# The low part of the values made ahead of the diagonal's sum, in a linear-attention and mixture-of-experts kernel

## The chip, the cores and the metric

The kernel runs on one core of a Trainium2 chip. Time is the device time of one execution in microseconds (us), as the median of some runs. The core's engines are TensorE (PE in the rows, its weight loads PEld), VectorE (DVE), ScalarE (ACT), GpSimd (POOL) and SyncE (SP), which here issues the DMAs. Each engine works through its own queue in order and meets the others at semaphores.

## The reference

Three stages follow each other: a linear attention with decay over 768 positions, a gated two-layer network, and a soft mixture of experts. Cut to what matters:

```python
for t in range(S):                                   # B, H, S, D = 4, 8, 768, 48
    cur = einsum('bhd,bhe->bhde', u[None] * k_t, v_t)
    y[:, :, t] = einsum('bhd,bhde->bhe', r_t, state + cur)
    state = w_t[..., None] * state + einsum('bhd,bhe->bhde', k_t, v_t)
x = y.transpose(0, 2, 1, 3).reshape(B * S, H * D)    # 3072 x 384
h = x @ w_in                                         # 384 -> 2048
x = (h * clip(h + 3, 0, 6) / 6) @ w_out
logits = x @ phi                                     # 32 slots
slots = softmax(logits over tokens).T @ x            # then 8 experts: relu(slots @ w1) @ w2
out = softmax(logits over slots) @ slots_out
```

## The kernel before

The attention is cut into 24 units of 128 positions: six chunks, and in each the four batches (unit n has batch n % 4). Within a unit the decayed sum over earlier positions of the same chunk is a masked product of scores and values, and what comes from earlier chunks goes through `state`. The term with `u` concerns each position alone: the sum over d of r * k * u for each of the 8 heads (`diag`, 128 x 8) times v.

The gated network runs over 96 steps: six groups of 512 tokens (one chunk of all batches) with 16 pieces of 128 hidden columns. A step s is nine matmuls of 128x512 in half precision on TensorE (`mlp`, L568 to L570), a relu on ScalarE (L1343), and on VectorE the gate (L997) and a transpose (L1018). `mlp(s)` needs gate s - 2. The steps are at the same time the clock of the attention: every unit has four of them, called phases 0 to 3, and `unit_of(s)` gives `divmod(s + 19, 4)`. The first five units are in part done ahead of the loop; units 5 to 23 have their phases in it. The order on each engine is written out by hand in that engine's loop, and nothing reorders it.

Values and scores are split into a high and a low half-precision part, so that TensorE can multiply them in half precision. For one unit n these are the pieces that matter here:

- ScalarE makes `v_hi` in phase 0 (`high_v`, L1273); VectorE makes `v_lo` = 64 * v - `v_hi` in phase 2 (`low_v`, L981, 128x384, both inputs in SBUF). TensorE's `attend` in phase 3 (L534 first, then L540 to L544) waits for it, and so does SyncE's load of the unit that takes the same buffer.
- GpSimd makes r * k * u in phase 0 (`diag_products`, L1494 and L1496); VectorE sums it by heads in phase 2 (`sum_diag`, L977, 128x384 to 128x8); GpSimd's `diag_values` (L1517) in phase 3 multiplies it with v, and `finish_y` (L955) on VectorE adds that to the output of `attend`. The next unit's `diag_products` waits for `diag_done` too.
- VectorE's `mask_scores` (L936) and `scan_suffix` (L904) in phase 1, `low_x` (L970) in phase 2 (for every fourth unit in phase 1), `scan_prefix` (L916) in phase 3. GpSimd's `low_scores` (L1523) in phase 1, `decay_keys` (L1532) in phase 2, `decay_receptance` (L1541) in phase 3, behind `scan_prefix`. TensorE's `score` (L470) in the next phase 0 needs both. In the first steps of the loop GpSimd also makes the low part of w_in (`low_w`, L1508), twice per unit in units 5 to 7.

On VectorE, phase 2 in the loop is followed by the gate and the transpose of the same step.

Of the kernel before, what the change touches and what calls it, by code (L numbers as in the profile page):

```python
# [48 lines left out]
def build_program(nc, wT, rkT, nat_in_dram, u, u_blocks, w_in, w_outT, w_out, phi, w1, w2, out):  # L49
    with ExitStack() as ctx:  # L50
# [14 lines left out]
        def pairs(ap, n):  # L65
            return ap.rearrange("p (i n) -> p i n", n=n)
# [88 lines left out]
        def nat_of(n, which):  # L155
            return nat_rows_of(n)[:, which * DM:(which + 1) * DM]
# [54 lines left out]
        def by_slot(ap):  # L211
            return ap.rearrange("p (i s) -> p i s", s=SLOTS)
# [128 lines left out]
        def unit_of(s):  # L341
            return divmod(s + 4 * B + 3, 4)

        def is_unit(n):
            return 0 <= n < UNITS
# [551 lines left out]
        def _(dve):  # L897
# [35 lines left out]
            def mask_scores(n):  # L933
                dve.wait_ge(scores_ready, 2 * n + 2)
                dve.wait_ge(scores_lo_done, n - B)
                nc.vector.tensor_tensor(scores.rearrange("p (o n) -> p o n", o=PB),  # L936
                                        sc_ps[:, :].rearrange("p (o n) -> p o n", o=PB),
                                        mask[:].rearrange("p (o n) -> p o n", o=1).broadcast_to([P, PB, 2 * P]),
                                        ALU.mult).then_inc(masked, 2)
# [10 lines left out]
            def finish_y(n):  # L950
                dve.wait_ge(y_ready, n + 1)
                dve.wait_ge(diag_v_done, n + 1)
                if n:
                    dve.wait_ge(x_turned, n)
                nc.vector.scalar_tensor_tensor(y_nat, y_ps[:, 0:DM], 1.0 / (Y_SCALE if n >= B else SCORE_SCALE), diag_v,  # L955
                                               ALU.mult, ALU.add)\
                    .then_inc(y_done, 1)

            def add_state(n):
                dve.wait_ge(inc_ready, 2 * n + 2)  # L960
                for j in range(2):
                    rows = slice(ALIGN * j, ALIGN * j + D)
                    s = state[n % B][rows, :, j * D:(j + 1) * D]
                    new = pairs(inc_ps[rows, 0:PB * 2 * D], 2 * D)[:, :, j * D:(j + 1) * D]
                    last = nc.vector.tensor_tensor(s, s, new, ALU.add)
                last.then_inc(state_added, 1)
# [6 lines left out]
            def sum_diag(n):  # L973
                dve.wait_ge(rku_done, n - B + 1)
                if n:
                    dve.wait_ge(diag_v_done, n)
                nc.vector.tensor_reduce(diag[:], pairs(rku, D), AX_X, ALU.add).then_inc(diag_done, 1)  # L977

            def low_v(n):
                dve.wait_ge(v_hi_done, n - B + 1)  # L980
                nc.vector.scalar_tensor_tensor(v_lo[n % 2], nat_of(n, 2), V_SCALE, v_hi[n % 2],  # L981
                                               ALU.mult, ALU.subtract).then_inc(v_lo_done, 1)
# [10 lines left out]
            def gate(s):  # L993
                dve.wait_ge(relu_done, s + 1)
                if s >= GATED:
                    dve.wait_ge(l_ready, 4 * ((s - GATED) // 4 + 1))
                nc.vector.scalar_tensor_tensor(gated_tile(s), relu_tile(s), 6.0 * GATE, hid[s % 2][:],  # L997
                                               ALU.min, ALU.mult).then_inc(gated_done, 1)
# [10 lines left out]
            def turn_gated(s):  # L1009
                g, i = divmod(s, FT)  # L1010
                dve.wait_ge(gated_done, s + 1)
                if s == STEPS - 1:
                    dve.wait_ge(late_gated_done, 1)
                if i >= 4 and g:
                    dve.wait_ge(dg_ready, 16 * g)
                elif g >= 2:
                    dve.wait_ge(dg_ready, 16 * (g - 1))
                nc.vector.transpose(ring_tile(s), gated_tile(s)).then_inc(gated_turned, 1)  # L1018
# [5 lines left out]
            def group_maximum(g):  # L1024
                dve.wait_ge(folded, g + 1)
                if g >= 2:
                    dve.wait_ge(alpha_done, g - 1)
                nc.vector.tensor_reduce(group_max, l_ps[:], AX_X, ALU.max).then_inc(group_max_done, 1)
                dve.wait_ge(group_max_done, g + 1)
                lower(group_max, g).then_inc(neg_max_done, 1)  # L1030
# [108 lines left out]
            for s in range(END):  # L1139
                n, phase = unit_of(s)  # L1140
                g, i = divmod(s, FT)
                if s <= 1:
                    gate(s)
                    if s == 0:
                        low_v(B)
                    turn_gated(s)
                if phase == 0:
                    if is_unit(n - 1):
                        finish_y(n - 1)
                    if n - 1 < LAST_INC:  # L1150
                        add_state(n - 1)
                if phase == 1:
                    if 1 <= g < C and i == 2:
                        group_maximum(g - 1)
                    if is_unit(n):
                        mask_scores(n)
                    if is_unit(n + 1):
                        scan_suffix(n + 1)
                        restart_prefix(n + 1)
                    if is_unit(n - 1) and n % B == 0 and n > B:  # L1160
                        low_x(n - 1)
                    if 1 <= g < C and i == 2:
                        if g == C - 1:
                            turn_gated(s - 1)
                        turn_weight(g - 1)
                        turn_logits(g - 1)
                    if g == C and i == 2:
                        last_maximum()
                if phase == 2:
                    if g == C and i == 3:  # L1170
                        turn_weight(C - 1)
                    if g >= 1 and i == 3:
                        sum_weight(g - 1)
                    if is_unit(n - 1) and n % B:
                        low_x(n - 1)
                    if is_unit(n):
                        sum_diag(n)
                        low_v(n)
                if s == 0:
                    sum_diag(B)  # L1180
                    low_w(1)
                if phase == 3:
                    if is_unit(n + 1) and n > B:
                        scan_prefix(n + 1)
                    if s == STEPS + 4:
                        dve.wait_ge(run_sum_done, C)
                        nc.vector.tensor_scalar(run_sum, run_sum, 1e-9, None, ALU.add).then_inc(sum_inv_step, 1)
                        dve.wait_ge(sum_inv_step, 1)
                        nc.vector.reciprocal(run_sum, run_sum).then_inc(sum_inv_step, 1)
                        dve.wait_ge(sum_inv_step, 2)  # L1190
                        nc.vector.tensor_scalar(fold_inv[:], fold32, run_sum, None, ALU.mult).then_inc(fold_inv_done, 1)
                        dve.wait_ge(fold_inv_done, 1)
                        nc.vector.tensor_scalar(fold_alpha, fold_inv[:], alpha, None, ALU.mult).then_inc(fold_inv_done, 1)
                    if 1 <= g < C and i == 4:
                        add_slots(g - 1)
                if s == 4:
                    dve.wait_ge(w_phi_ready, 4)
                    nc.vector.transpose(w_phi[:], l_ps[:]).then_inc(w_phi_done, 1)
                if s == STEPS - 12:
                    cols, tiles = c_parts[0]  # L1200
                    dve.wait_ge(logits_done, C - 1)
                    nc.vector.tensor_reduce(cmax[:, tiles], by_slot(soft[:, cols]), AX_X, ALU.max).then_inc(c_max_done, 1)
                if s == STEPS - 8:
                    c_inverse(0)
                if s == STEPS + 3:
                    copy_cT(1)
                    copy_cT(0)
                if 1 < s < STEPS - 1:
                    gate(s)
                if 1 < s < STEPS - 2 and s != STEPS - FT + 1:  # L1210
                    turn_gated(s)
                if s == STEPS - 1:
                    last_gate(0)
                    turn_gated(STEPS - 2)
                    last_gate(1)
                    turn_gated(STEPS - 1)
# [462 lines left out]
```

## Time and profile before

| | us |
|---|---|
| median of 3 runs (lowest to highest) | 422.92 (421.85 to 425.69) |
| profiled execution, its own time | 421.91 |
| its span | 420.2 |
| VectorE busy in it | 338.0 |
| GpSimd busy in it | 187.7 |

The span is the time from the first to the last instruction of the profiled execution; its own time has what lies around that as well. TensorE's granted clock was 0.992 of full speed in the mean. A start time in a row counts from the span's start. TensorE's matmuls are pipelined and overlap, so that one which is listed with 0.38 us is followed by the next after 0.22.

### The profile page before, as it was taken

What the parts mean: (1) busy time and instruction counts of PE and PEld (TensorE: products, weight loads), DVE (VectorE), ACT (ScalarE), POOL (GpSimd) and SP (SyncE); (2) the same over time, 40 slices, a digit from 0 to 9 for tenths busy, and PEclk for the clock granted to TensorE, in tenths of its full rate; (3) what the DMA queues carried; (4) which work ended last, traced back from release to release, by engine and by line L of the source; (5) the groups of instructions that cost most, each with busy time, mean ns of one, the idle gap of its engine ahead of it and who ended that gap; (6) DMA issues with size and microseconds to landing.
All of it is one profiled execution on the core that took longest, in us unless ns stands there. A gap on an engine that the chain in (4) does not pass through costs nothing.

```text
span 420.2 us, 9784 instructions
## 1 busy us (share of the span) xinstructions
PE 402.2 (96%) x3914; PEld 220.2 (52%) x3914; DVE 338.0 (80%) x559; ACT 162.3 (39%) x297; POOL 187.7 (45%) x178
## 2 busy tenths in 40 slices
PE   8999999999999999999999999989999999999981
PEld 3884555555555555555555555445553444543430
DVE  7998799998998988989989988989875787661151
ACT  3586256534334244244343333341433234421141
POOL 4445988874555654455744557454540012010000
PEclk9999999999999999999999999999999999999996
DMA  8998331368034213304340331231007099879929
GB/s 245 354 400 277 123 96 29 123 264 274 11 122 122 80 48 123 116 9 123 124 123 2 123 120 51 77 123 58 0 4 297 4 367 411 247 272 420 386 97 357
DMA packets 16397, 69.35 MB, mean 165 GB/s; under 512 B 2144, under 2 KB 2912, under 8 KB 14688
## 3 DMA queue, kind: packets, MB, share of 16 engines
q1 hardware_dynamic: 16352, 68.73, 46.5%
q8 instruction: 31, 0.51, 0.5%
q14 instruction: 14, 0.11, 0.1%
HBM read 64.00 MB, written 4.72 MB: 164 GB/s over the span
## 4 chain that ended last, share of the span: by engine, by line
issue 35%; PE 29%; POOL 22%; DMA 5%; DVE 4%; ACT 1%; POOLq 0%; SPq 0%; DVEq 0%
POOL att L1532 5%; PE hid L568 4%; PE hid L570 4%; DMA att<-rkT_dram 4%; PE hid L569 4%; POOL att L1494 4%; POOL att L1496 4%; POOL att L1517 3%; POOL att L1550 3%; POOL w_split L1508 3%; PE hid L834 3%; PE l_ps L675 2%; PE hid L815 1%; PE sc_ps L815 1%; PE l_ps L615 1%
## 5 line engine op out<-in xcount | busy, mean ns | idle before, releaser
L1343 ACT ACTIVATE relu<-hid,three 128x512 f32<-128x512 f32 x95 | 65.2, 686 | 138.0 <-PE hid L570 137.7
L568 PE MATMUL hid<-x_split,w_split 128*128 128x512 f16 x285 | 108.3, 380 | 0.4 <-DVE gated L997 0.4
L570 PE MATMUL hid<-x_split,w_split 128*128 128x512 f16 x285 | 108.0, 379 | 0.0
L569 PE MATMUL hid<-x_split,w_split 128*128 128x512 f16 x285 | 108.0, 379 | 0.0
L997 DVE SCALAR_TENSOR_TENSOR gated<-relu,hid 128x512 f32<-128x512 f32 x95 | 64.4, 678 | 22.8 <-ACT relu L1343 22.1
L1018 DVE STREAM_TRANSPOSE ring<-gated 128x512 f32<-128x512 f32 x96 | 68.3, 711 | 3.3
L1523 POOL TENSOR_TENSOR att<-att 128x1024 f16<-128x1024 f32 x20 | 40.9, 2045 | 48.4 <-ACT att L1278 48.4
L1541 POOL TENSOR_TENSOR att<-att 112x512 f32<-112x512 f32 x19 | 23.2, 1220 | 57.0 <-DVE att L916 57.0
L568 PEld LDWEIGHTS hid<-x_split,w_split 128*128 128x128 f16 x285 | 27.7, 97 | 36.8 <-DVE gated L997 6.3
L570 PEld LDWEIGHTS hid<-x_split,w_split 128*128 128x128 f16 x285 | 27.8, 98 | 33.7
L569 PEld LDWEIGHTS hid<-x_split,w_split 128*128 128x128 f16 x285 | 27.9, 98 | 25.0 <-issue 0.3
L534 PE MATMUL y_ps<-att 112*128 112x96 f32 x160 | 33.6, 294 | 2.0 <-DVE att L981 1.4
L1532 POOL TENSOR_TENSOR att<-att 112x512 f32<-112x512 f32 x21 | 25.8, 1229 | 9.6 <-DVE att L904 9.6
L470 PEld LDWEIGHTS sc_ps<-att 48*128 48x128 f32 x384 | 23.3, 187 | 10.7 <-issue 10.7
L904 DVE TENSOR_TENSOR_SCAN att<-att 112x517 f32<-112x517 f32 x22 | 27.9, 1269 | 1.2 <-DMA att<-wT_dram 1.2
L916 DVE TENSOR_TENSOR_SCAN att<-att 112x517 f32<-112x517 f32 x22 | 28.2, 1284 | 0.0
L534 PEld LDWEIGHTS y_ps<-att 112*128 112x128 f32 x160 | 24.9, 189 | 6.4 <-issue 4.6
L470 PE MATMUL sc_ps<-att 48*128 48x128 f32 x384 | 27.9, 284 | 0.0
L1301 ACT ACTIVATE x_split<-y_ps 128x384 f16<-128x384 f32 x24 | 11.8, 491 | 41.1 <-PE y_ps L551 41.1
L675 PE MATMUL l_ps<-ring,soft 32*32 32x512 f32 x192 | 25.4, 593 | 2.3 <-DVE logits L1037 1.5
L675 PE MATMUL sc_ps<-ring,soft 32*32 32x512 f32 x384 | 26.1, 598 | 0.0
L1278 ACT ACTIVATE att<-att 128x1024 f16<-128x1024 f32 x20 | 21.1, 1057 | 11.6 <-DVE att L936 10.9
(269 smaller groups left out, 757.7 us busy)
## 6 DMA issues: line engine op xcount, KB each, us to landing
att<-nat_dram SPq DMA_DIRECT2D x20, 576.0 KB, 4.0
att<-rkT_dram SPq DMA_DIRECT2D x22, 448.0 KB, 5.5
att<-wT_dram SPq DMA_DIRECT2D x22, 226.2 KB, 4.7
att<-w_dram SPq DMA_DIRECT2D x3, 1536.0 KB, 10.0
out_dram<-w_split SPq DMA_DIRECT2D x12, 384.0 KB, 3.9
att<-w_dram SPq DMA_DIRECT2D x5, 768.0 KB, 9.9
stage<-w_in_dram SPq DMA_DIRECT2D x2, 1536.0 KB, 13.6
ring<-w_outT_dram SPq DMA_DIRECT2D x1, 3072.0 KB, 15.2
```

Of the source, the lines that this page charges most:

```text
L470: last = pe.matmul(sc_bank[j][:, cols], k_dec[n % 2][rows, cols], r_dec[n % 2][rows, cols], start=True, stop=True)
L534: pe.matmul(both, r_dec[n % 2][0:PD, p * P:(p + 1) * P], state[b][0:PD, p, :], start=True, stop=False, skip_group_check=True)
L568: pe.matmul(hid[s % 2][:], high, x_high, start=(q == 0), stop=False)
L569: pe.matmul(hid[s % 2][:], high, x_low, start=False, stop=False)
L570: last = pe.matmul(hid[s % 2][:], low, x_high, start=False, stop=(q == KT - 1))
L675: ins = pe.matmul(dg_bank[a][SLOTS * c:SLOTS * (c + 1), :], weight_T[SLOTS * a:SLOTS * (a + 1), b * SLOTS:(b + 1) * SLOTS], ring_group(g, ...
L916: nc.vector.tensor_tensor_scan(prefix[0:PD, :], w_rows_of(n)[0:PD, :], restart[0:PD, :], 1.0, ALU.mult, ALU.add).then_inc(prefix_done, 1)
L997: nc.vector.scalar_tensor_tensor(gated_tile(s), relu_tile(s), 6.0 * GATE, hid[s % 2][:], ALU.min, ALU.mult).then_inc(gated_done, 1)
L1018: nc.vector.transpose(ring_tile(s), gated_tile(s)).then_inc(gated_turned, 1)
L1343: nc.scalar.activation(relu_tile(s), hid[s % 2][:], ACT.Relu, bias=three[:], scale=GATE / H_SCALE)\
L1523: nc.gpsimd.tensor_tensor(scores_lo, scores, scores_hi, ALU.subtract).then_inc(scores_lo_done, 1)
L1532: nc.gpsimd.tensor_tensor(dst, keys, decay, ALU.mult).then_inc(k_dec_done, 1)
```

## The change

In phase 2 of each unit of the loop, on VectorE, `low_v(n)` stands ahead of `sum_diag(n)` in place of behind it. Both functions, their waits and their signals are as before. The unit whose pair lies ahead of the loop's phase 2 (unit 4) is not touched.

```diff
                     if is_unit(n - 1) and n % B:
                         low_x(n - 1)
                     if is_unit(n):
+                        low_v(n)
                         sum_diag(n)
-                        low_v(n)
                 if s == 0:
                     sum_diag(B)
```

On VectorE in phase 2 of unit 6, between the transpose of the step before and the next `scan_prefix` (L970 is `low_x`, L977 `sum_diag`, L981 `low_v`, L997 the gate, L1018 the transpose, L916 `scan_prefix`). Before:

```order
L970 SCALAR_TENSOR_TENSOR x_split<-y_ps,x_split 128x3x128
L977 TENSOR_REDUCE diag<-att 128x8
L981 SCALAR_TENSOR_TENSOR att<-att 128x384
L997 SCALAR_TENSOR_TENSOR gated<-relu,hid 128x512
L1018 STREAM_TRANSPOSE ring<-gated 128x512
L916 SCALAR_TENSOR_TENSOR att<-att 112x517
```

And in the changed kernel:

```order
L970 SCALAR_TENSOR_TENSOR x_split<-y_ps,x_split 128x3x128
L981 SCALAR_TENSOR_TENSOR att<-att 128x384
L977 TENSOR_REDUCE diag<-att 128x8
L997 SCALAR_TENSOR_TENSOR gated<-relu,hid 128x512
L1018 STREAM_TRANSPOSE ring<-gated 128x512
L916 SCALAR_TENSOR_TENSOR att<-att 112x517
```

`low_v` now follows `low_x`, and `sum_diag` stands between it and the gate.

In a unit whose number is a multiple of four (here unit 8) `low_x` is further ahead, in phase 1, and the pair follows a gate and a transpose (L936 `mask_scores`, L904 `scan_suffix`, L909 a reciprocal). Before:

```order
L936 TENSOR_TENSOR att<-sc_ps,mask 128x1024
L904 SCALAR_TENSOR_TENSOR att<-att 112x517
L909 RECIPROCAL att<-att 112x4
L970 SCALAR_TENSOR_TENSOR x_split<-y_ps,x_split 128x3x128
L997 SCALAR_TENSOR_TENSOR gated<-relu,hid 128x512
L1018 STREAM_TRANSPOSE ring<-gated 128x512
L977 TENSOR_REDUCE diag<-att 128x8
L981 SCALAR_TENSOR_TENSOR att<-att 128x384
L997 SCALAR_TENSOR_TENSOR gated<-relu,hid 128x512
```

And in the changed kernel:

```order
L936 TENSOR_TENSOR att<-sc_ps,mask 128x1024
L904 SCALAR_TENSOR_TENSOR att<-att 112x517
L909 RECIPROCAL att<-att 112x4
L970 SCALAR_TENSOR_TENSOR x_split<-y_ps,x_split 128x3x128
L997 SCALAR_TENSOR_TENSOR gated<-relu,hid 128x512
L1018 STREAM_TRANSPOSE ring<-gated 128x512
L981 SCALAR_TENSOR_TENSOR att<-att 128x384
L977 TENSOR_REDUCE diag<-att 128x8
L997 SCALAR_TENSOR_TENSOR gated<-relu,hid 128x512
```

`low_v` here comes straight behind the transpose. The queues of TensorE, ScalarE, GpSimd and SyncE are the same in both kernels.

## Rows read from the trace of the kernel before

**Rows 1.** The page's head: span; busy us (share of the span) xinstructions.
```profile
span 420.2 us, 9784 instructions
PE 402.2 (96%) x3914; PEld 220.2 (52%) x3914; DVE 338.0 (80%) x559; ACT 162.3 (39%) x297; POOL 187.7 (45%) x178
```

**Rows 2.** Lines L981 and L977 by source: shortest/median/longest ns, first to last start.
```profile
L981 DVE SCALAR_TENSOR_TENSOR att<-att x20: 543/706/1440, 39.6 to 311.0; 128x384 f16<-128x384 f32 x20
L977 DVE TENSOR_REDUCE diag<-att x20: 504/532/544, 40.9 to 310.5; 128x8 f32<-128x384 f32 x20
```

**Rows 3.** Waits: who <- for whom: us in total, times, longest.
```profile
DVE gated L997 <- ACT relu L1343: 22.1, 26, 1.8
...
PE y_ps L534 <- DVE att L981: 1.4, 3, 0.5
```

**Rows 4.** Timeline, unit 6, VectorE, GpSimd, TensorE: start, us, what [idle before].
```profile
66.21 0.53 DVE L977 TENSOR_REDUCE diag<-att 128x8 f32<-128x384 f32 x1
66.66 1.44 DVE L981 SCALAR_TENSOR_TENSOR att<-att 128x384 f16<-128x384 f32 x1
68.03 0.67 DVE L997 SCALAR_TENSOR_TENSOR gated<-relu,hid 128x512 f32<-128x512 f32 x1
...
69.37 1.19 DVE L916 TENSOR_TENSOR_SCAN att<-att 112x517 f32<-112x517 f32 x1
...
63.77 2.32 POOL L1523 TENSOR_TENSOR att<-att 128x1024 f16<-128x1024 f32 x1 [0.56 <-ACT att L1278]
66.05 1.64 POOL L1508 TENSOR_TENSOR w_split<-stage,w_split 128x768 f16<-128x768 f32 x1
67.65 1.50 POOL L1532 TENSOR_TENSOR att<-att 112x512 f32<-112x512 f32 x1
...
68.36 0.43 PE L534 MATMUL y_ps<-att 112*128 112x96 f32 x2 [0.48 <-DVE att L981]
```

**Rows 5.** Timeline, unit 15, the same engines.
```profile
196.15 0.71 DVE L981 SCALAR_TENSOR_TENSOR att<-att 128x384 f16<-128x384 f32 x1
...
195.26 1.19 POOL L1532 TENSOR_TENSOR att<-att 112x512 f32<-112x512 f32 x1
...
197.95 0.36 PE L534 MATMUL y_ps<-att 112*128 112x96 f32 x2
```

**Rows 6.** Timeline from unit 6's phase 3 to unit 7's.
```profile
70.64 1.19 POOL L1541 TENSOR_TENSOR att<-att 112x512 f32<-112x512 f32 x1 [1.50 <-DVE att L916]
...
72.11 0.38 PE L470 MATMUL sc_ps<-att 48*128 48x128 f32 x2
...
72.71 0.56 DVE L955 SCALAR_TENSOR_TENSOR att<-y_ps,att 128x384 f32<-128x384 f32 x1 [0.82 <-POOL att L1517]
...
75.28 1.19 DVE L936 TENSOR_TENSOR att<-sc_ps,mask 128x1024 f32<-128x1024 f32 x1
...
77.64 2.31 POOL L1523 TENSOR_TENSOR att<-att 128x1024 f16<-128x1024 f32 x1 [0.57 <-ACT att L1278]
...
83.23 1.19 DVE L916 TENSOR_TENSOR_SCAN att<-att 112x517 f32<-112x517 f32 x1
```

**Rows 7.** Timeline, unit 20, VectorE, GpSimd, TensorE.
```profile
266.95 0.51 DVE L977 TENSOR_REDUCE diag<-att 128x8 f32<-128x384 f32 x1
267.38 1.23 DVE L981 SCALAR_TENSOR_TENSOR att<-att 128x384 f16<-128x384 f32 x1
...
265.06 2.00 POOL L1523 TENSOR_TENSOR att<-att 128x1024 f16<-128x1024 f32 x1 [2.53 <-ACT att L1278]
267.02 1.18 POOL L1532 TENSOR_TENSOR att<-att 112x512 f32<-112x512 f32 x1
...
266.43 0.38 PE L568 MATMUL hid<-x_split,w_split 128*128 128x512 f16 x1 [0.42 <-DVE gated L997]
...
268.87 0.32 PE L534 MATMUL y_ps<-att 112*128 112x96 f32 x1 [0.34 <-DVE att L981]
```

## Prediction

> **What bounds the kernel now.** I read the page's head first: TensorE is busy for 402.2 of the 420.2 us of the span, VectorE for 338.0 [rows 1]. The change touches two VectorE instructions of a unit and no other, so the list of waits comes next: does TensorE ever wait for one of them? It waited for `low_v` (L981) three times, 1.4 us in all [rows 3], and never for `sum_diag` (L977). The same list says that VectorE waited 26 times, 22.1 us in all, for ScalarE's relu, which itself waits for TensorE's products: in many steps VectorE has air, and a small delay of it dies at the next relu. So what counts is where it has none. I went through the loop unit by unit in the order of time and laid VectorE, GpSimd and TensorE side by side.
>
> What the reader is to see there is the length of `low_v`. It does the same work 20 times, and takes 543 ns at least, 706 in the median and 1440 at most, while `sum_diag` stays between 504 and 544 [rows 2]. In unit 6 `low_v` starts at 66.66 and ends at 68.10; GpSimd's L1508 runs beside it and ends at 67.69, so `low_v` ends 0.41 us behind it. GpSimd's L1532, which starts at 67.65, takes 1.50 us there, against 1.19 in unit 15 [rows 4, 5]. In unit 15 `low_v` starts at 196.15, L1532 ends at 195.26 + 1.19 = 196.45, and `low_v` ends at 196.86, again 0.41 behind. In unit 20: L1532 ends at 268.20, `low_v` at 268.61, the same 0.41 [rows 7]. So `low_v` doesn't run slowly beside these GpSimd instructions, it doesn't run at all until they end; one that is waiting is let in before GpSimd's next. `sum_diag`, at 66.21 to 66.74 in the middle of L1508, is not held up.
>
> The Trainium skill says why, in "SBUF — State Buffer", section "Who interferes with whom": a VectorE instruction with both inputs in SBUF shares a port with GpSimd instructions that read SBUF, and the one that issues second blocks fully until the first is through; a reduction never does. By that rule `sum_diag` is a free filler ahead of a blocked `low_v`, and the rule speaks against the change; were it bandwidth that is shared, the order would not matter and the sum would be zero. The trace agrees with the rule: 0.41 us behind the end of GpSimd's instruction, three times over.
>
> **The change, step by step.** Nothing is added or removed; two neighbours trade places in the 19 units 5 to 23. From one's start to the other's (66.21 to 66.66) is 0.45 us, which I take for `sum_diag`'s length in the queue.
>
> Step 1, where GpSimd holds the port. Unit 6: `low_v` now asks at 66.21 in place of 66.66. L1523 ended at 63.77 + 2.32 = 66.09, L1508 has the port until 67.69; `low_v` still ends at 68.10. `sum_diag`, hidden under L1508 before, now comes behind, and the gate (L997, 68.03) starts 0.45 us later. VectorE loses 0.45 us, `low_v` gains nothing. By the same reading of the timeline this holds in 14 of the 19 units; in the other five (9, 13, 17, 21 and 23) GpSimd is silent and the swap costs nothing on VectorE.
>
> Step 2, who is behind VectorE. In units 5 to 7 the following ring closes: gate, transpose, `scan_prefix` (L916, 69.37), GpSimd's `decay_receptance` (L1541, from 70.64, ends at 71.83) and `diag_values`, `finish_y` (L955, which waited 0.82 for it), gate, `mask_scores` (L936, 75.28), ScalarE's copy of the scores, GpSimd's `low_scores` (L1523, 77.64), its second L1508, `low_v`, and `scan_prefix` again at 83.23 [rows 6]. No relu wait stands in it, and one turn is 83.23 - 69.37 = 13.86 us. There 0.45 is lost in each of units 5, 6 and 7: 1.35 us. TensorE feels it through L470, the scores, which need L1541: it started at 72.11, 0.28 us behind L1541's end. 1.35 - 0.28 = 1.07 us. The wait for `low_v` (0.48 in unit 6 [rows 4]) grows with the ring, and is no second term.
>
> Step 3, the quiet units (10 to 18). In unit 15 TensorE's `attend` (L534) starts at 197.95, and `low_v` was done at 196.86: 1.1 us of slack [rows 5]. That `v_lo` comes sooner buys nothing, and a gate that is 0.45 late is caught by the relu waits [rows 3]: 22.1 / 26 = 0.85 us in the mean. I take zero. If that cover were gone, each unit would cost 0.45.
>
> Step 4, the units of a multiple of four. Here `low_x` stands further ahead, and `low_v` follows the transpose. Unit 20: the first of the pair starts at 266.95, and L1523 holds the port until 265.06 + 2.00 = 267.06, L1532 comes at 267.02 [rows 7]. By 0.11 us `low_v` would ask while L1523 still runs, get in before L1532, and end near 267.06 + 0.41 = 267.47 instead of 268.61: VectorE gains 268.61 - 267.47 - 0.45 = 0.7 us. A tenth of a microsecond decides, so both ends stay: in unit 8, behind the ring, winning costs no more and losing carries another 0.45 to TensorE. In unit 20 TensorE has already waited 0.42 for a gate and 0.34 for `low_v` [rows 7], so the 0.45 that unit 19 loses arrives whole; a win here gives back 0.34 of it, and a loss nothing: +0.1 to +0.45.
>
> GpSimd's own queue: `diag_values` waits for `diag_done`, and what stands behind it there (`decay_state`, `diag_products`) would wait as well. In unit 6 `sum_diag` would end near 68.10 + 0.45, and L1541, which stands ahead of `diag_values`, started at 70.64: 2 us to spare. Only unit 23 has no L1541 ahead; there `finish_y`, the one that is waited for, comes behind TensorE's `attend` and not behind `diag_values`. SyncE's loads wait for `v_lo_done`, which comes no later. Zero for all three.
>
> Sum: 1.07 (step 2) + 0 to 0.45 (unit 8) + 0.1 to 0.45 (unit 20) = 1.2 to 2.0; I take 1.6, the middle, since the two coin-flips stand alone. The profiled execution took 421.91 us (span 420.2); it becomes 423.5. It lies 1.0 under the median of the three runs, 422.92, to which my number is made: 422.92 + 1.6 = 424.5. A change of less than 1% of it, 4.2 us, is about what a measurement of this kernel can't tell from none.
>
> **The rivals.**
> A, all is absorbed. For it: the 22.1 us of relu waits, and that TensorE's work per unit hardly leaves holes. Against: the ring has no relu wait. 422.9.
>
> B, `low_v` wins the port. In unit 6 it misses L1523's end by 66.21 - 66.09 = 0.12 us. Were it to win there too, TensorE's three waits for `low_v` would go, 1.4 us [rows 3]; behind that stands TensorE's own queue, so no more. 422.9 - 1.4 = 421.5. For it: the margin is small, and a VectorE that lags no longer waits for relu, and so comes to the port relatively sooner. Against: in the ring nothing changes the relative times of L1523 and `low_v`, as both follow from L936.
>
> C, the slower side: the lag accumulates. If the quiet units had no air and each of the 14 blocked `low_v` cost TensorE 0.45 us, the time would be 422.9 + 6.3 = 429.2. It decides from the point at which VectorE's lag exceeds the 1.1 us between `low_v` and `attend`, or the relu waits, so after three units in a row without one. Against: the first relu wait resets it, and a won port gives 0.7 back.
>
> D, that the swap doesn't do what it says: both instructions have had their inputs for microseconds (ScalarE's `high_v` and GpSimd's products run two steps before), so neither holds the other up. I see no way for this.
>
> **How the numbers follow.** My forecast (slower by 1.2 to 2.0 us) 0.52; A 0.22; B 0.19; C 0.06; something unseen 0.01. The range reaches from B to the forecast's upper end, and a little over, since the three runs of before lie from 1.1 under to 2.8 over their median: 421.2 to 426.6. It leaves out C. Slower by over 1%: C and a rest, 0.07; faster by over 1%: 0.02, as nothing here gives 4.2 us; within 1%: 0.91.
>
> **What would show it.** Right: `low_v`'s median goes up from 706 ns by some 0.45 us, since it asks sooner, while it ends no sooner in units 5 to 7; `scan_prefix` starts there follow each other in about 14.3 us instead of 13.86; the waits of TensorE for `low_v` grow in units 6 and 7; from unit 9 on all is shifted by 1 to 1.6 us. Step 4: in units 8, 12, 16 and 20 `low_v` ends 0.41 us behind L1523 and L1532 is longer by 0.3. It is wrong if the ring's turn stays at 13.86 us (then A), if `low_v` ends before L1508 in units 6 and 7 (then B), or if the relu waits vanish (C).

## The result, and the profile after

The changed kernel takes 423.68 us in the median of 20 runs, the kernel before, run beside it, 422.28: the ratio is 1.0038, with a 95% interval of 1.0019 to 1.0056. The medians differ by 1.40 us; the ratio, taken over fast runs and so without one of the changed kernel at 431.27 us, makes it 1.6 us (0.8 to 2.4). That is less than 1%, but clear of the measurement's own scatter. The forecast was 1.6 us. (That it named 424.5 in place of 423.7 comes for 0.64 us from the median of before, which was 422.92 over three runs and is 422.28 over twenty, and for the rest from 1.6 against 1.40.)

The page's head of the changed kernel; it answers to [rows 1]:

```profile
span 421.7 us, 9784 instructions
PE 402.7 (95%) x3914; PEld 220.7 (52%) x3914; DVE 340.4 (81%) x559; ACT 161.8 (38%) x297; POOL 188.5 (45%) x178
```

The same number of instructions; VectorE is busy 2.4 us longer. Where that is, the views by source of the two exchanged lines show (shortest/median/longest in ns), and the list of waits beside them; they answer to [rows 2] and [rows 3]:

```profile
L981 DVE SCALAR_TENSOR_TENSOR att<-att x20: 518/824/1890, 39.5 to 312.3; 128x384 f16<-128x384 f32 x20
L977 DVE TENSOR_REDUCE diag<-att x20: 505/540/549, 40.8 to 312.8; 128x8 f32<-128x384 f32 x20
```

```profile
DVE gated L997 <- ACT relu L1343: 21.5, 26, 1.7
...
PE y_ps L534 <- DVE att L981: 1.5, 2, 0.7
...
PE hid L568 <- DVE gated L997: 0.9, 1, 0.9
```

`sum_diag` (L977) is about as long as it was (median 540 against 532 ns), though it has moved. `low_v` (L981) is longer at the long end, 1.89 us against 1.44, and shorter at the short one. Both ends have their place in the timeline. Unit 6, which answers to [rows 4], with the same order of engines:

```profile
66.56 1.89 DVE L981 SCALAR_TENSOR_TENSOR att<-att 128x384 f16<-128x384 f32 x1
68.38 0.54 DVE L977 TENSOR_REDUCE diag<-att 128x8 f32<-128x384 f32 x1
68.84 0.67 DVE L997 SCALAR_TENSOR_TENSOR gated<-relu,hid 128x512 f32<-128x512 f32 x1
70.18 1.19 DVE L916 TENSOR_TENSOR_SCAN att<-att 112x517 f32<-112x517 f32 x1
...
64.14 2.31 POOL L1523 TENSOR_TENSOR att<-att 128x1024 f16<-128x1024 f32 x1 [0.58 <-ACT att L1278]
66.40 1.64 POOL L1508 TENSOR_TENSOR w_split<-stage,w_split 128x768 f16<-128x768 f32 x1
68.00 1.50 POOL L1532 TENSOR_TENSOR att<-att 112x512 f32<-112x512 f32 x1
...
68.71 0.43 PE L534 MATMUL y_ps<-att 112*128 112x96 f32 x2 [0.73 <-DVE att L981]
```

`low_v` asks at 66.56, 0.11 us after L1523's end (64.14 + 2.31 = 66.45), L1508 has the port until 68.04, and `low_v` ends at 68.45, 0.41 behind it. `sum_diag`, which was hidden under L1508 in [rows 4], now starts when `low_v` ends, and the gate behind it. The ring goes on as in [rows 6]:

```profile
71.45 1.18 POOL L1541 TENSOR_TENSOR att<-att 112x512 f32<-112x512 f32 x1 [1.96 <-DVE att L916]
...
72.74 1.16 PE L470 MATMUL sc_ps<-att 48*128 48x128 f32 x16 [0.20 <-issue]
...
84.50 1.19 DVE L916 TENSOR_TENSOR_SCAN att<-att 112x517 f32<-112x517 f32 x1
```

From one `scan_prefix` (L916) to the next it is 84.50 - 70.18 = 14.32 us, and was 13.86. The scores (L470) now start 0.11 us behind GpSimd's L1541 (72.63), and TensorE waits for it, where before it came 0.28 us behind L1541 and did not wait.

The other end of `low_v`'s lengths is in unit 20, which answers to [rows 7]:

```profile
268.95 0.52 DVE L981 SCALAR_TENSOR_TENSOR att<-att 128x384 f16<-128x384 f32 x1
269.39 0.54 DVE L977 TENSOR_REDUCE diag<-att 128x8 f32<-128x384 f32 x1
...
267.06 2.00 POOL L1523 TENSOR_TENSOR att<-att 128x1024 f16<-128x1024 f32 x1 [2.54 <-ACT att L1278]
269.01 1.49 POOL L1532 TENSOR_TENSOR att<-att 112x512 f32<-112x512 f32 x1
...
268.43 0.38 PE L568 MATMUL hid<-x_split,w_split 128*128 128x512 f16 x1 [0.90 <-DVE gated L997]
270.36 0.36 PE L534 MATMUL y_ps<-att 112*128 112x96 f32 x2
```

`low_v` asks at 268.95, while L1523 still runs (to 269.06), and gets in ahead of L1532, which now takes 1.49 us in place of 1.18: the port is won. TensorE no longer waits for `low_v` there, but it waits 0.90 us for a gate, where it waited 0.42: VectorE came into this unit late. Its first matmul of the step (L568) is 268.43 - 266.43 = 2.00 us later than before, and `attend` only 270.36 - 268.87 = 1.49.

And the quiet unit 15, which answers to [rows 5]:

```profile
197.17 1.22 DVE L981 SCALAR_TENSOR_TENSOR att<-att 128x384 f16<-128x384 f32 x1
...
196.80 1.18 POOL L1532 TENSOR_TENSOR att<-att 112x512 f32<-112x512 f32 x1
...
199.03 0.36 PE L534 MATMUL y_ps<-att 112*128 112x96 f32 x2
```

TensorE is 199.03 - 197.95 = 1.08 us later than before, as it has been since unit 8; `low_v` ends at 198.39 against 196.86, 1.53 later. The 1.09 us between `low_v` and `attend` have shrunk to 0.64, without being used up. (Where TensorE waits for `low_v`, 0.26 us are left between them, as in [rows 4]; the room in unit 15 was thus 0.83 us, and 0.38 is left.)

A second place is narrower. The scores of the next unit (L470) need GpSimd's L1541, which follows `scan_prefix`. For unit 16, before:

```profile
199.40 1.18 POOL L1541 TENSOR_TENSOR att<-att 112x512 f32<-112x512 f32 x1 [2.95 <-DVE att L916]
...
201.63 1.16 PE L470 MATMUL sc_ps<-att 48*128 48x128 f32 x16
```

And in the changed kernel:

```profile
201.39 1.18 POOL L1541 TENSOR_TENSOR att<-att 112x512 f32<-112x512 f32 x1 [3.41 <-DVE att L916]
...
202.71 1.16 PE L470 MATMUL sc_ps<-att 48*128 48x128 f32 x16
```

L470 came 1.05 us behind L1541's end, and comes 0.14 behind it now; where TensorE waits for L1541, as ahead of the scores of units 7 and 8, it is 0.10.

To see where time goes, take the start of TensorE's first L534 in a unit (`attend`), subtract the same of the kernel before, and subtract what the two traces differ by in unit 4, ahead of the change (a few values are 0.01 or 0.02 off by rounding). All kernels of the next section are in the table, except three whose profiled execution took 2 to 3 us more than their median and lost them up to unit 5, before the loop's first `mask_scores` (us, later than before):

| | unit 6 | unit 7 | unit 8 | unit 18 | unit 20 | unit 23 |
|---|---|---|---|---|---|---|
| changed kernel | 0.45 | 0.90 | 1.18 | 1.18 | 1.59 | 1.65 |
| swap in 5 to 7 | 0.46 | 0.90 | 1.30 | 1.38 | 1.40 | 1.41 |
| swap from 8 on | 0.02 | 0.01 | 0.02 | 0.02 | 0.45 | 0.51 |
| filler ahead, 5 to 7 | 0.02 | 0.02 | 0.03 | 0.03 | -0.30 | -0.29 |
| filler behind, 5 to 7 | 0.46 | 0.93 | 1.32 | 1.40 | 1.07 | 1.08 |
| swap in 8, 12, 16, 20 | 0.00 | -0.01 | 0.00 | 0.00 | -0.50 | -0.58 |
| second piece of w_in later | 2.27 | 3.40 | 3.41 | 3.42 | 3.41 | 3.42 |
| low_v first, piece later | -0.65 | -1.43 | -1.17 | -1.16 | -2.08 | -1.56 |
| one memset | 0.01 | -0.01 | 0.00 | 0.00 | -0.33 | -0.32 |
| changed, quiet filler | 0.46 | 0.91 | 1.18 | 3.32 | 4.20 | 4.27 |

For the changed kernel: 1.18 us from units 5 to 7, nothing in the ten units up to 18, and 0.41 in units 19 and 20 (0.11 of it in unit 19).

### The profile page after: what moved, and what is told of

Same layout as the page of the kernel before. It is cut to its first block, busy times and chain, and to the rows that moved or that the text cites. A ratio compares the mean times of both kernels' runs of the same rounds, so it can differ in the third digit from the quotient of the medians.

```text
span 421.7 us, 9784 instructions
## 1 busy us (share of the span) xinstructions
PE 402.7 (95%) x3914; PEld 220.7 (52%) x3914; DVE 340.4 (81%) x559; ACT 161.8 (38%) x297; POOL 188.5 (45%) x178
## 4 chain that ended last, share of the span: by engine, by line
issue 35%; PE 30%; POOL 22%; DMA 5%; DVE 4%; ACT 1%; POOLq 0%; SPq 0%; DVEq 0%
POOL att L1532 5%; PE hid L568 4%; PE hid L570 4%; PE hid L569 4%; DMA att<-rkT_dram 4%; POOL att L1494 4%; POOL att L1496 4%; POOL att L1517 3%; POOL att L1550 3%; POOL w_split L1508 3%; PE hid L834 3%; PE l_ps L675 2%; PE hid L815 1%; PE sc_ps L815 1%; PE l_ps L615 1%
## 5 line engine op out<-in xcount | busy, mean ns | idle before, releaser
L568 PE MATMUL hid<-x_split,w_split 128*128 128x512 f16 x285 | 108.3, 380 | 0.9 <-DVE gated L997 0.9
L997 DVE SCALAR_TENSOR_TENSOR gated<-relu,hid 128x512 f32<-128x512 f32 x95 | 64.4, 678 | 22.1 <-ACT relu L1343 21.5
L1018 DVE STREAM_TRANSPOSE ring<-gated 128x512 f32<-128x512 f32 x96 | 68.3, 711 | 3.3
L1523 POOL TENSOR_TENSOR att<-att 128x1024 f16<-128x1024 f32 x20 | 40.9, 2044 | 48.6 <-ACT att L1278 48.6
L1541 POOL TENSOR_TENSOR att<-att 112x512 f32<-112x512 f32 x19 | 23.2, 1219 | 57.5 <-DVE att L916 57.5
L568 PEld LDWEIGHTS hid<-x_split,w_split 128*128 128x128 f16 x285 | 27.7, 97 | 37.4 <-DVE gated L997 7.3
L534 PE MATMUL y_ps<-att 112*128 112x96 f32 x160 | 33.6, 294 | 2.1 <-DVE att L981 1.5
L1532 POOL TENSOR_TENSOR att<-att 112x512 f32<-112x512 f32 x21 | 27.1, 1289 | 9.6 <-DVE att L904 9.6
L470 PEld LDWEIGHTS sc_ps<-att 48*128 48x128 f32 x384 | 23.5, 187 | 11.8 <-issue 11.8
L904 DVE TENSOR_TENSOR_SCAN att<-att 112x517 f32<-112x517 f32 x22 | 27.9, 1270 | 1.1 <-DMA att<-wT_dram 1.1
L470 PE MATMUL sc_ps<-att 48*128 48x128 f32 x384 | 27.9, 283 | 0.9 <-issue 0.8
L916 DVE TENSOR_TENSOR_SCAN att<-att 112x517 f32<-112x517 f32 x22 | 28.3, 1284 | 0.0
L534 PEld LDWEIGHTS y_ps<-att 112*128 112x128 f32 x160 | 25.1, 189 | 6.0 <-issue 4.0
```

Source lines behind the costliest of these rows:

```text
L470: last = pe.matmul(sc_bank[j][:, cols], k_dec[n % 2][rows, cols], r_dec[n % 2][rows, cols], start=True, stop=True)
L534: pe.matmul(both, r_dec[n % 2][0:PD, p * P:(p + 1) * P], state[b][0:PD, p, :], start=True, stop=False, skip_group_check=True)
L568: pe.matmul(hid[s % 2][:], high, x_high, start=(q == 0), stop=False)
L916: nc.vector.tensor_tensor_scan(prefix[0:PD, :], w_rows_of(n)[0:PD, :], restart[0:PD, :], 1.0, ALU.mult, ALU.add).then_inc(prefix_done, 1)
L1523: nc.gpsimd.tensor_tensor(scores_lo, scores, scores_hi, ALU.subtract).then_inc(scores_lo_done, 1)
L1532: nc.gpsimd.tensor_tensor(dst, keys, decay, ALU.mult).then_inc(k_dec_done, 1)
```

## The experiments

Medians and ratios are against runs of the kernel before on the same chip.

### The two halves of the change

```diff
 # e1_swap_5_7; in e2_swap_8_on: if n >= 8
                     if is_unit(n):
-                        sum_diag(n)
-                        low_v(n)
+                        if n < 8:
+                            low_v(n)
+                            sum_diag(n)
+                        else:
+                            sum_diag(n)
+                            low_v(n)
```

> The two trade places in units 5, 6 and 7 alone. Theory (the ring of those units, in which GpSimd's L1508 holds low_v up): most of the cost is here, +1.1 us over the kernel before, starts of scan_prefix 14.3 us apart, and nothing after unit 8. Rival (each of the 14 held-up low_v costs the same): 3/14 of 1.5 us, +0.3. Rival (the measured difference is noise or the placing of the code): 0.

> The two trade places in units 8 to 23 alone. Theory: TensorE has the slack to hide it up to unit 18, and loses 0.3 to 0.5 us in units 19 and 20, so +0.4 us in all, with low_v let in ahead of L1532 in units 8, 12, 16 and 20. Rival (the same price everywhere): 11/14 of 1.5, +1.2.

Units 5 to 7 alone: 423.54 against 422.18 us, ratio 1.0045 (1.0011 to 1.0078). Units 8 on alone: 422.61 against 422.18, 1.0017 (0.9991 to 1.0043). In the first, `scan_prefix` starts at 56.12, 70.43 and 84.74, a ring of 14.31 us, and TensorE is 1.38 us late from unit 9 on. In the second TensorE loses nothing up to unit 18 and 0.45 by unit 20; the timed difference has 1 in its interval, the trace's is plain. So neither is the price spread evenly over the 14 held-up `low_v`, nor is it noise. That the first half alone costs a little more than in the full change (1.38 against 1.18) is unit 8: there the full change wins the port, and in the half, which has the old order in unit 8, `low_v` ends 0.26 us before `attend`, as where TensorE waits for it, so that the whole lag of VectorE (1.37 us) arrives at TensorE.

### Is it the place behind low_v, or just 0.45 us of VectorE?

One more reduction in units 5 to 7, of the same size, whose output nobody reads:

```diff
+            def filler():
+                nc.vector.tensor_reduce(stats[:, 64:72], pairs(u_all, D), AX_X, ALU.add)
...
                         sum_diag(n)
+                        if n < 8:        # e3_filler_ahead
+                            filler()
                         low_v(n)
+                        if n < 8:        # e4_filler_behind, instead
+                            filler()
```

> The order of before, and in units 5 to 7 one more reduction of the same size (of u, into unused columns) between sum_diag and low_v. Theory (low_v can't begin before L1508 ends, so what stands ahead of it is hidden): low_v ends when it did, +0.0 to 0.1 us. Rival (in that ring any 0.45 us of VectorE costs 0.45, wherever it stands): +1.1.

> The same added reduction in units 5 to 7, but behind low_v; sum_diag and its signal stand where they were. Theory: as dear as the swap, +1.1 us, ring of 14.3 us. Rival (the swap costs because diag_done comes 1.8 us later and GpSimd waits for it): 0, since diag_done isn't later here.

Ahead: 421.78 against 422.18 us, ratio 0.9977 (0.9952 to 1.0001). Behind: 423.53 against 422.18, 1.0028 (0.9995 to 1.006). The timeline of the first, VectorE and GpSimd in unit 6 (L980 is the filler, L984 `low_v`, L1513 what was L1508):

```profile
66.35 0.53 DVE L977 TENSOR_REDUCE diag<-att 128x8 f32<-128x384 f32 x1
66.81 0.54 DVE L980 TENSOR_REDUCE stats<-att 128x8 f32<-128x384 f32 x1
67.26 0.99 DVE L984 SCALAR_TENSOR_TENSOR att<-att 128x384 f16<-128x384 f32 x1
...
66.19 1.64 POOL L1513 TENSOR_TENSOR w_split<-stage,w_split 128x768 f16<-128x768 f32 x1
```

The reader is to add: `low_v` starts 0.45 us later than it would and is 0.45 shorter (0.99 against 1.44 in [rows 4]); it ends at 68.25, and L1513 at 67.83, 0.42 before. TensorE is 0.03 us late at unit 8, where the same reduction behind `low_v` makes it 1.32 late (1.40 by unit 18), with a ring of 14.31 us (`scan_prefix` at 56.20 and 70.51). Timed, the interval of the second still holds 1, but each of its runs (422.97 us or more) lies above each of the first (422.07 or less). That both kernels gain 0.33 us by unit 20 has another cause, which the last experiment takes up. Whether it is also why the kernel with the filler ahead is timed below the one of before is not shown; the kernels with memsets, which gain the same in the trace, are not timed below it. The second kernel also has `diag_done` where it was, and costs as much as the swap: that `sum_diag` signals GpSimd later is not what costs.

### Where the port is won

```diff
                     if is_unit(n):
+                        if n % B == 0:   # low_v first here, the old order in the others
```

> The two trade places in units 8, 12, 16 and 20 alone, where the changed kernel's low_v was let in ahead of L1532. Theory: VectorE gains some 0.7 us in each, TensorE uses only what it waited in unit 20: -0.3 us. Rival (a swap costs wherever it is): +0.2 to 0.4.

421.56 against 422.09 us, ratio 0.9983 (0.9949 to 1.0017). In the trace TensorE gains nothing in units 8 to 18, and 0.50 us at unit 20; `low_v` takes 0.52 us in unit 8, where it took 1.22. The sign is as expected; the timing alone can't tell it from nothing. The size is 0.50 and not 0.34, because the wait of TensorE that goes is longer than listed: the 0.34 of [rows 7] count from the end of a matmul of 0.38 us that the next could have followed after 0.22, and with these 0.16 it is 0.50.

The port was not won in all four. In unit 12 it was lost (L1527 and L1536 are what was L1523 and L1532):

```profile
148.54 2.00 POOL L1527 TENSOR_TENSOR att<-att 128x1024 f16<-128x1024 f32 x1 [2.18 <-ACT att L1282]
150.50 1.18 POOL L1536 TENSOR_TENSOR att<-att 112x512 f32<-112x512 f32 x1
...
150.65 1.45 DVE L981 SCALAR_TENSOR_TENSOR att<-att 128x384 f16<-128x384 f32 x1
```

`low_v` asks 0.11 us behind L1527's end (150.54) and takes 1.45 us, and VectorE loses 0.46 instead of gaining 0.7. In the changed kernel it asks 0.11 us before that end in the same unit, since VectorE comes there with a lag and so doesn't stand for 0.13 us ahead of the gate (149.13 in the kernel before), until ScalarE's relu has ended (149.10). TensorE loses nothing by it: a later wait for a relu takes it up. So the tenth of a microsecond does decide, and a lag from the units ahead shifts it.

So what if it won in units 5 to 7 too? `low_v` ahead of `low_x` too asks 0.45 us sooner:

```diff
+                    if is_unit(n):
+                        low_v(n)
                     if is_unit(n - 1) and n % B:
                         low_x(n - 1)
                     if is_unit(n):
                         sum_diag(n)
-                        low_v(n)
```

> low_v stands ahead of low_x as well, in all units: it asks for the port 0.45 us sooner than in the changed kernel, in unit 6 at about 65.8, before L1523 ends at 66.1. Theory: it is let in at L1523's end, ends near 66.5 in place of 68.1, VectorE gains 0.65 us (1.6 less low_x and sum_diag, which now come behind), L1508 and L1532 shift by 0.3; TensorE's 1.4 us of waits for low_v go: -1.4 us. Rival (GpSimd's next instruction keeps the port, or low_x 0.4 us later holds TensorE up): low_v ends behind L1508, and two instructions lie behind it: +1.5 to 2.

420.43 against 422.09 us, ratio 0.9962 (0.9945 to 0.998): 1.7 us faster than before. It is the only kernel here whose interval stays below 1. Its profiled execution is none to read the start of: it took 423.49 us, 3 more than the median. VectorE is 3.2 us late at the loop's first `mask_scores`: half of that arose ahead of the loop and in its first steps, beginning with a wait of 0.74 us for a DMA, and half in one stop just ahead of it:

```profile
49.64 1.23 DVE L936 TENSOR_TENSOR att<-sc_ps,mask 128x1024 f32<-128x1024 f32 x1 [1.88 <-issue]
```

Nothing shown releases it; the kernel before has 0.32 us of it. How `low_v` comes through in this order is read from a kernel that has it too.

### Moving what low_v waits for

In units 5 to 7 GpSimd makes two pieces of w_in's low part. The second goes behind `decay_keys` (L1532):

```diff
-            return {1: 2, 2: 3, 5: 4, 6: 5, 9: 6, 10: 7}.get(s)
+            return {1: 2, 3: 3, 5: 4, 7: 5, 9: 6, 11: 7}.get(s)
```

> The order of before on VectorE; in units 5 to 7 GpSimd makes the second piece of w_in's low part behind decay_keys (L1532) instead of ahead of it. Then it is L1532 (1.18 us) that holds low_v up and not L1508 (1.64). Theory: low_v ends 0.45 us sooner in each of the three units, the ring's turn goes from 13.86 to 13.4, and TensorE saves some 1.0 us until it is the bound itself. Rival (L1508, now at the time of scan_prefix, blocks that one instead): 0.

> low_v first of all (as in the kernel that has only this) and the second piece behind L1532. Theory: both point to the same wait, and it is gone with the first: -1.4 us, no more than low_v first alone, or worse by up to 0.5 if L1508 now meets scan_prefix. Rival (the ring is still what bounds, and both count): -2 to -2.5.

The piece later, by itself: 425.82 against 422.09 us, ratio 1.0088 (1.0063 to 1.0113). Neither theory nor rival; it is 3.7 us slower. Its timeline in unit 5, VectorE, GpSimd and TensorE:

```profile
53.11 2.37 DVE L981 SCALAR_TENSOR_TENSOR att<-att 128x384 f16<-128x384 f32 x1
...
52.28 1.18 POOL L1532 TENSOR_TENSOR att<-att 112x512 f32<-112x512 f32 x1
53.42 1.64 POOL L1508 TENSOR_TENSOR w_split<-stage,w_split 128x768 f16<-128x768 f32 x1
...
55.74 0.43 PE L534 MATMUL y_ps<-att 112*128 112x96 f32 x2 [0.84 <-DVE att L981]
```

`low_v` asks at 53.11, L1532 ends at 53.46, and then GpSimd's next has the port first: `low_v` ends at 55.48, 0.42 behind L1508 (55.06). It lost twice. In units 6 and 7 it takes 2.58 us in the same way. My step from [rows 4], that a `low_v` which waits is let in before GpSimd's next, held for the pair L1508 to L1532 and not for L1532 to L1508. That the loss per unit is the one more instruction fits: TensorE is 1.00, 2.26 and 3.40 us later in units 5, 6 and 7.

Both together: 420.82 against 422.09 us, ratio 0.9978 (0.9951 to 1.0004). Unit 6 in it (L1524 and L1533 are what was L1523 and L1532):

```profile
65.90 0.73 DVE L981 SCALAR_TENSOR_TENSOR att<-att 128x384 f16<-128x384 f32 x1
...
68.83 1.54 DVE L916 TENSOR_TENSOR_SCAN att<-att 112x517 f32<-112x517 f32 x1
...
63.92 2.31 POOL L1524 TENSOR_TENSOR att<-att 128x1024 f16<-128x1024 f32 x1 [0.57 <-ACT att L1279]
66.18 1.49 POOL L1533 TENSOR_TENSOR att<-att 112x512 f32<-112x512 f32 x1
```

`low_v` comes in at L1524's end (66.23) and is done at 66.63; the ring turns in 82.36 - 68.83 = 13.53 us. `scan_prefix`, with two inputs in SBUF as well, now meets the moved piece, and takes 1.54 us in place of 1.19. With `low_v` first alone it takes 1.54 too, beside GpSimd's `decay_keys`, and the ring turns in 13.5 us. Counted from unit 5 on, so behind its late start, TensorE in that kernel gains 0.65 us by unit 6, 1.43 by unit 7, 1.17 by unit 18 and 1.59 by unit 23, as here. So moving the piece adds nothing to `low_v` first, as the theory had it, and takes nothing back that a trace shows; the medians differ by 0.4 us. The port isn't won everywhere in either: in units 10, 15 and 22 `low_v` takes 1.39 to 1.45 us beside L1533.

### How much room the quiet units have

```diff
                         low_v(n)
                         sum_diag(n)
+                        if 10 <= n <= 18:
+                            filler()
```

> The changed kernel, and in the quiet units 10 to 18 one more reduction behind sum_diag, so that VectorE has 0.45 us more in each. In the changed kernel VectorE's lag there reached 0.9 of the 1.1 us between low_v and attend. Theory (TensorE is hidden from VectorE by that slack alone): it is used up in the second or third unit of each group, and units 10 to 18 cost 0.4 to 2 us more. Rival (TensorE is the bound with far more room): 0.

426.17 against 422.01 us, ratio 1.0111 (1.007 to 1.0151): 4.2 us slower than before, so some 2.6 more than the changed kernel, which was not run beside it. In the trace TensorE is 1.18 us late up to unit 11 and 3.32 at unit 18: 2.1 us for nine added reductions of 0.45 in units 10 to 18. From there to unit 20 it loses 0.88, where the changed kernel loses 0.41. In unit 15 (L984 is `low_v`):

```profile
198.92 1.22 DVE L984 SCALAR_TENSOR_TENSOR att<-att 128x384 f16<-128x384 f32 x1
...
200.39 0.43 PE L534 MATMUL y_ps<-att 112*128 112x96 f32 x2
```

`low_v` ends at 200.14, 0.25 before `attend`, as in [rows 4], where TensorE waits: the slack is gone. But `attend` is not where TensorE loses most. Its longest stops are ahead of the scores of the next unit, which need GpSimd's L1546 (what was L1541):

```profile
203.60 1.18 POOL L1546 TENSOR_TENSOR att<-att 112x512 f32<-112x512 f32 x1 [3.88 <-DVE att L916]
...
204.88 1.16 PE L470 MATMUL sc_ps<-att 48*128 48x128 f32 x16 [0.66 <-issue]
```

From L1541's end to L470, by the unit of the scores (us):

| | 11 | 12 | 15 | 16 | 19 | 20 |
|---|---|---|---|---|---|---|
| kernel before | 1.23 | 1.22 | 1.06 | 1.06 | 0.57 | 0.57 |
| changed kernel | 0.80 | 0.33 | 0.60 | 0.14 | 0.11 | 0.10 |
| changed, quiet filler | 0.34 | 0.10 | 0.10 | 0.10 | 0.10 | 0.10 |

With the filler TensorE stands 0.61 us ahead of the scores of unit 12, 0.35 of unit 15 and 0.66 of units 16 and 19. I expected 0.4 to 2 us for units 10 to 18, and it is 2.1, with the slack between `low_v` and `attend` as the reason, where it is mostly that between L1541 and L470. In the changed kernel two losses of 0.45 in a row add up there, and only 0.04 us of room is left for the scores of unit 16.

### The hitch ahead of unit 19's finish_y

In the trace of before, and in all of the first ten but the two with a filler, VectorE starts `finish_y` of unit 19 0.44 us behind `diag_values`, where it is 0.09 in each other unit in which that is what it waits for:

```profile
260.14 0.56 DVE L955 SCALAR_TENSOR_TENSOR att<-y_ps,att 128x384 f32<-128x384 f32 x1 [1.17 <-POOL att L1517]
```

```diff
                     if is_unit(n - 1):
+                        if n == 8:
+                            for q in range(1):   # 3 in e10_three_memsets
+                                nc.vector.memset(stats[:, 64 + q:65 + q], 0.0)
                         finish_y(n - 1)
```

> The kernel before with one tiny memset on VectorE (one unused column) just ahead of finish_y of unit 7, where VectorE waits anyway. It is for the 0.35 us for which VectorE stood before finish_y of unit 19 in every kernel but the two with three added instructions. Theory (a hitch in the supply of VectorE's instructions, at a fixed count of them): it moves to another instruction, still in unit 19, and the time stays within 0.2 us or falls by 0.3. Rival (an event of unit 19 itself): still 0.44 us between diag_values' end and finish_y.

> The same with three memsets. Theory of the count: no hitch before finish_y of unit 19, as in the kernels with three added reductions, and -0.3 to -0.5 us. Rival: the hitch stays, 0.

> low_v ahead of low_x in all units, with the three memsets. Theory: -1.7 us from the order, as measured, and up to -0.3 from the hitch that is gone: -1.7 to -2.0; in its profile a ring of 13.5 us and no wait of TensorE for low_v in units 5 to 8. Rival (the profile of that order, in which VectorE stood for 1.9 us before the first mask_scores of the loop, is typical of it): the hole again, and nothing gained in the profile's span.

With one memset:

```profile
260.56 0.56 DVE L955 SCALAR_TENSOR_TENSOR att<-y_ps,att 128x384 f32<-128x384 f32 x1 [0.81 <-POOL att L1520]
```

The hitch is gone, and TensorE is 0.33 us early at unit 20, with one memset and with three (there counted from unit 5). So it isn't an event of unit 19 itself. In the eight traces that have it, it stands before VectorE's 371st instruction, and every kernel with instructions added ahead of that place lacks it. So the count of instructions may be what matters, but the hitch was not found at another instruction of unit 19, where the theory had it move. And the timed medians don't follow: 422.04 and 422.03 against 422.01 us, ratios 0.9996 (0.9976 to 1.0016) and 1.0025 (0.9997 to 1.0053); the fastest runs are the same too (421.58 and 421.56 against 421.61). Whether the hitch is a cost of ordinary runs, or moves to another place ahead of the loop, stays open. The profiled executions can't say, as both were late ahead of the change's place, by 0.75 us in unit 4 with one memset and by 2.6 in unit 5 with three. With `low_v` first: 420.24 against 422.01, 0.9974 (0.9946 to 1.0003), again 1.8 us faster in the medians, and with the 1.9 us stop in its profiled execution (423.51 us) once more; the ring in it turns in 13.54 us, and TensorE doesn't wait for `low_v` in units 5 to 8, as expected. Of the twelve and nine runs of the two kernels with `low_v` first two and three took over 422.5 us, the profiled ones among them, and the others 420.05 to 421.25. The kernel with three memsets and the order of before has a stop of 1.55 us at the same place in its profiled execution, and the one with `low_v` first and the piece later only 0.33: the stop belongs to some runs, not to the order.

## Why the prediction was right

Step 1, the port: right in units 5 to 7, to the hundredth. `low_v` ended 0.41 us behind L1508 and not sooner, `sum_diag` came out from under it, and the ring's turn grew from 13.86 to 14.32 where 14.3 was said. The fillers bear it out: three times 0.45 us ahead of `low_v` cost 0.03 by unit 8, behind it 1.32. Of the 14 units in which I had VectorE lose 0.45, it lost in ten and won the port in four.

Step 2, 1.07 us through L470: TensorE was 0.90 late at unit 7's `attend` and 1.18 at unit 8's. The term is right within 0.11, and that is the 0.28 taken off: TensorE follows L1541 by 0.10 even where it waits for it, so only 0.18 was room (the ring's lag of 1.37 less 0.19 is 1.18). The first half alone gives 1.38, of which unit 8, with its old order, is the last part.

Step 3, zero in the quiet units: right, and in part by luck. VectorE was 1.53 us later in unit 15 and TensorE 1.08, so at `attend` 0.45 of 0.83 us of room was used. But the step looked for room there alone. Two blocked units in a row add up before anything resets the lag, and for the scores of unit 16 it had 0.92 of the 0.96 us (1.06 less 0.10) between L1541 and L470: 0.04 us more, and quiet units would have cost. With twice the delay they did, 2.1 us. Rival C was the right one to fear: its mechanism works, after two units in a row and not three, and one more 0.45 per unit brings it in.

Step 4, the units of a multiple of four: the port was won in all four (0.52 us in units 8, 12, 16 and 20), so unit 8 carried nothing on. In unit 20 I had counted 0.1 for a won port and 0.45 for a lost one; it was won, and cost 0.41 (1.18 to 1.59). This is the term that was mis-sized: I took the lag that enters unit 20 for the 0.45 of unit 19 alone. But VectorE's `scan_prefix` in unit 19's phase 3 started at 258.45 against 256.46, 1.99 us later, where TensorE was 1.08 later up to unit 18: 0.91, the loss of unit 18 as well. And a won port gives back 0.50 and not 0.34, since the listed wait leaves out a part of it, as the swap in the fours shows: 0.91 - 0.50 = 0.41, as measured. Unit 8 was put too high by half of 0.45, unit 20 too low by 0.13 and the ring by 0.11. These errors cancel, which is luck, and the sum came out right: 1.65 in the trace, 1.4 to 1.6 timed.

Of the signs that I named, one was wrong: the median of `low_v` rose from 706 to 824 ns only, not by 0.45 us, since the four won ports joined the five silent units at the short end.

Rival B, the port won in units 5 to 7, is real as a state of this kernel: `low_v` 0.45 us earlier still makes it, and gives 1.7 us where 1.4 was worked out from the three waits. That the two lie so near is partly chance: in the trace with the piece later TensorE gains 1.43 by unit 7 already, stands at 1.17 up to unit 18, and ends at 1.56 after 2.08 at unit 20. The change moved `low_v` by just 0.1 us too little for it there.

## What to carry to other kernels

An engine that stands behind another's port has free time ahead of the blocked instruction and none behind it: look for instructions of equal work whose length varies (0.54 to 1.44 us here), see what ends 0.4 us before they do, and put unrelated work ahead of them. Or move the blocked instruction far enough that it asks before the other engine's next instruction starts; moving it a little less than that, 0.1 us here, is worse than not moving it. (With L1508 behind L1532 asking before the next one's start wasn't enough.) A delay on an engine off the path is free only up to its slack, and the slack has to be followed over several units, where each adds its own, and on every path from that engine to the bound one: here the nearer wait, `attend`, had 0.38 us left where the scores had 0.04.

## What the runs showed of the hardware

Which of the two waiting engines gets the port at the end of a GpSimd instruction is not simply who asked first. In the ten traces of the kernel before, the changed one and the first eight experiments a `low_v` that waited was let in ahead of GpSimd's next instruction, where one followed at once, 61 times (L1496, L1508 or L1523 ended), and three times it was not: all three at the end of an L1532 with L1508 next, though in unit 5 `low_v` had asked 0.31 us before L1508's start. Why that pair is different wasn't tried.

VectorE stood for 0.35 us before its 371st instruction in the eight of those ten traces that have the same number of VectorE instructions, and a single tiny instruction added 12 units earlier took that away. What causes it is open, and so is whether ordinary runs have it.
